# Expert products two units ahead: the order of first products, weight parts and relu in a decay attention and mixture-of-experts kernel

## The reference

```
out = decayed linear attention of q, k, v          # (2, 8, 768, 64)
x   = out as 1536 tokens of 512 features
e   = argmax(x @ w_gate);  gate = softmax(...)[e]
for each expert e, for its own tokens xe:
    y = gate * (relu(xe @ w1[e]) @ w2[e])
h = y @ w_in;  result = (h - tanh(h)) @ w_out
```

## Time and profile before

| | |
|---|---|
| median of 3 runs | 547.7 us (543.15 to 550.82) |
| profiled execution | 547.09 us, span 545.2 us, mean TensorE clock 0.983 |
| TensorE busy | 509.8 us, 94% of the span |
| VectorE, ScalarE, GpSimd busy | 367.3, 257.4, 319.4 us |
| chain that ended last | TensorE 85%, VectorE 4%, DMA 4%, issue 3%, ScalarE 2%, GpSimd 1% |
| DMA | 64.55 MB, mean 118 GB/s |

### The profile page before, as it was taken

One profiled execution on the slowest core, in us unless ns is written; L12 is line 12 of the kernel. 1 busy time (PEld: TensorE's weight loads), 2 busy tenths in 40 slices (PEclk: granted clock), 3 DMA queues, 4 the chain that ended last, 5 costly groups with the idle time before them and its releaser, 6 DMA issues.

```text
span 545.2 us, 10842 instructions
## 1 busy us (share of the span) xinstructions
PE 509.8 (94%) x3948; PEld 452.5 (83%) x3949; DVE 367.3 (67%) x513; ACT 257.4 (47%) x467; POOL 319.4 (59%) x263
## 2 busy tenths in 40 slices
PE   5999748799999999999999999999999999999994
PEld 4899648799999999999888888888888888888883
DVE  7333266756546455364379999989987774998781
ACT  1222316466656566476455454545444434443431
POOL 4766046635454444445368988986855554875553
PEclk9999969899999999999999999999999999999998
DMA  8878426465667757767280000000100000100002
GB/s 312 319 274 291 164 66 200 155 204 175 234 206 215 232 189 231 215 206 232 74 298 1 1 0 1 1 1 20 59 0 1 1 1 0 60 20 1 0 1 77
DMA packets 32410, 64.55 MB, mean 118 GB/s; under 512 B 3697, under 2 KB 7793, under 8 KB 32369
## 3 DMA queue, kind: packets, MB, share of 16 engines
q1 hardware_dynamic: 30448, 57.71, 32.2%
q0 software_dynamic: 1920, 6.29, 3.5%
HBM read 57.69 MB, written 6.29 MB: 117 GB/s over the span
## 4 chain that ended last, share of the span: by engine, by line
PE 85%; DVE 4%; DMA 4%; issue 3%; ACT 2%; POOL 1%; SPq 1%; ACTq 0%; DVEq 0%; POOLq 0%
PE bank L318 25%; PE bank L320 25%; PE bank L319 24%; DMA wst<-in_w_dram 3%; PE bank L1156 2%; PE bank L1131 2%; PE bank L1142 2%; PE bank L1178 1%; PE bank L1242 1%; PE bank L1185 1%; PE bank L1168 1%; DVE x_sorted L1031 1%; POOL out_dram L650 1%; ACT x_h L742 1%; DMA x_sorted<-token_rows,tokid 1%
## 5 line engine op out<-in xcount | busy, mean ns | idle before, releaser
L608 POOL TENSOR_TENSOR w_l<-wst,w_h 128x512 fp32r<-128x512 f32 x64 | 84.5, 1321 | 105.7 <-ACT w_h L713 105.7
L658 POOL TENSOR_SCALAR big<-h_sq 128x512 uint8<-128x512 f32 x48 | 80.3, 1673 | 37.3 <-ACT h_sq L797 37.0
L671 POOL TENSOR_TENSOR g_l<-g,g_h 128x512 fp32r<-128x512 f32 x48 | 63.9, 1330 | 45.5 <-ACT g_h L807 45.5
L318 PE MATMUL bank<-wo_h,g_h 128*128 128x512 f32 x192 | 75.4, 393 | 0.0
L320 PE MATMUL bank<-wo_l,g_h 128*128 128x512 f32 x192 | 75.1, 391 | 0.0
L319 PE MATMUL bank<-wo_h,g_l 128*128 128x512 f32 x192 | 74.6, 389 | 0.0
L320 PE MATMUL bank<-x_l,win_h 128*128 128x512 f32 x188 | 74.3, 395 | 0.0
L318 PE MATMUL bank<-x_h,win_h 128*128 128x512 f32 x188 | 73.9, 393 | 0.0
L319 PE MATMUL bank<-x_h,win_l 128*128 128x512 f32 x188 | 73.7, 392 | 0.0
L318 PE MATMUL bank<-xs_h,w_h 128*128 (+1 forms) x256 | 70.9, 277 | 2.6 <-issue 1.4
L318 PE MATMUL bank<-h_h,w_h 128*128 128x232 f32 x256 | 71.6, 280 | 1.5 <-DVE h_l L1021 1.3
(11 more groups left out here) (159 smaller groups left out, 1098.5 us busy)
## 6 DMA issues: line engine op xcount, KB each, us to landing
wst<-in_w_dram SPq DMA_DIRECT2D x128, 256.0 KB, 3.9
qk_in<-in_qk_t_dram SPq DMA_DIRECT2D x12, 512.0 KB, 6.1
kv_in<-in_kv_dram SPq DMA_DIRECT2D x12, 512.0 KB, 5.2
win<-in_w_in_dram SPq DMA_DIRECT2D x8, 512.0 KB, 4.5
wo<-in_w_out_dram SPq DMA_DIRECT2D x8, 512.0 KB, 8.0
token_rows<-x_sb SPq DMA_DIRECT2D x12, 256.0 KB, 3.4
x_sorted<-token_rows,tokid POOLq DMA_INDIRECT x12, 4.6
out_dram<-rows,tokid POOLq DMA_INDIRECT x12, 3.0
```

Of the source, the lines that this page charges most:

```text
L318: pe.matmul(dst, lh, rh, start=start, stop=False, skip_group_check=True)
L608: pool.tensor_tensor(w2_l[:, j % STG], wst2[:, j % STG], w2_h[:, j % 2].bitcast(F32), ALU.subtract).then_inc(w2l_ready, 1)
L658: pool.tensor_scalar(big[:, f % 2], h_sq[:, f % 2], T * T, None, ALU.is_ge).then_inc(big_ready, 1)
L671: pool.tensor_tensor(g_l[:, f % 2], g[:, f % 2], g_h[:, f % 2].bitcast(F32), ALU.subtract).then_inc(gl_ready, 1)
```

## The change

TensorE now runs F two units ahead: F(0) and F(1) come before the loop, and at each j the order is F(j+2), then in expert 0 the tiles of that j, then S(j). At j = 6 and 7 F belongs to the next expert, and the wait for all tiles and pads of expert 0 stands at j = 6.

On ScalarE the high part of w1 comes ahead of relu, with a wait for F(j) of its own. relu waits also for S(j-2), which read the h_h buffer. On VectorE the low part of w1 comes ahead of h_l. Tiles 2 to 11 are spread over six values of j: (2, 3), (4, 5), (6), (7, 8), (9, 10), (11); before over seven: (2, 3), (4), (5, 6), (7), (8, 9), (10), (11).

```diff
-    LATER = [[t for t in range(2, NT) if (t - 2) * (JT - 1) // (NT - 2) == j] for j in range(JT)]
+    LATER = [[t for t in range(2, NT) if (t - 2) * (JT - 2) // (NT - 2) == j] for j in range(JT)]
...
             def hidden(j, unit):
                 act.wait_ge(first_done, unit + 1)
+                ge(act, second_done, unit - 1)
                 act.activation(h_h[:, j % 2], bank[:, j % 4, 0:WIN], ACT.Relu).then_inc(hh_ready, 1)
...
                 for j in range(JT):
                     unit = JT * e + j
+                    if not (last and j + 2 >= JT):
+                        act.wait_ge(first_done, unit + 1)
+                        w1_high(j + 2, unit + 2, arrived(e, j + 2))
                     hidden(j, unit)
                     if first:
                         scale(LATER[j])
-                    if not (last and j + 2 >= JT):
-                        w1_high(j + 2, unit + 2, arrived(e, j + 2))
...
                     unit = JT * e + j
+                    if not (last and j + 2 >= JT):
+                        w1_low(j + 2, unit + 2)
                     hidden(j, unit)
                     if first:
                         scale(LATER[j])
-                    if not (last and j + 2 >= JT):
-                        w1_low(j + 2, unit + 2)
...
                 for j in range(JT):
-                    if j + 1 < JT:
-                        first_product(off, j + 1, JT * e + j + 1)
+                    if j + 2 < JT:
+                        first_product(off, j + 2, JT * e + j + 2)
                     elif not last:
-                        if first:
-                            pe.wait_ge(xsl_ready, NT)
-                            pe.wait_ge(pad_ready, 2)
-                        first_product(offset(e + 1), 0, JT * e + JT)
+                        if j + 2 == JT:
+                            if first:
+                                pe.wait_ge(xsl_ready, NT)
+                                pe.wait_ge(pad_ready, 2)
+                            off = offset(e + 1)
+                        first_product(off, j + 2 - JT, JT * e + j + 2)
...
             first_product(0, 0, 0)
+            first_product(0, 1, 1)
```

## The result

The changed kernel takes 576.65 us (median of 4 runs, 573.15 to 585.57), the kernel before 548.23 in the same comparison. The ratio is 1.057 (95% interval 1.050 to 1.063): slower. Ratios here leave out executions in the chip's slower state, such as the one of 585.57. The forecast was 571, with a range from 558 to 584.

The account below looks back on a forecast made before the run. TensorE was taken to bound the expert and last stages. Losses of 14.7, 10.8, 2.1, 1.0 and 1.2 us, less 1.6 and 4.4, gave +23.8 on 547.09: 571 us, range 558 to 584.

Parts of the forecast that it names:

- What bounds it: Expert and last stages are both set by TensorE, so only its gaps can be won; the last stage is untouched.
- The 4.4 us: Gaps at j = 1 and 2 in six later experts, from relu queued behind w1's DMA wait: all 4.4 us won.
- Term 1: F of j = 3, experts 1 to 7: w1's load behind win's comes about 2.1 us late each, 14.7 us.
- Term 2: F of j = 6 (expert 0: j = 7): win_l ahead of w1's low part, 1.35 each, 10.8 us.
- Term 4: The end: S(63) late because w2's high part waits for S(61) with one product as cover, 1.0 us.
- Term 3: GpSimd's w2 low part holds VectorE's w1 low part: 0.1 us at three units in each of seven experts, 2.1 us.
- Restarts: TensorE's slower product behind each of 15 new gaps, 0.08 us each, 1.2 us.
- Term 5: Expert 0: tile 8's wait and slow clock shrink, two late units cost 0.85 each; -1.6 us, between -4.5 and +1.5.
- The clock: Rival: the clock falls at the seven 2 us gaps, adding 11 us, so 582 us; 12 in 100.
- Rival 1: The gap is paid once, not in every expert, since later loads run far enough ahead: 546 us; 7 in 100.
- Rival 2: Either win_l's delay or the load's delay behind win hides, the other not: 560 or 564 us; 18 in 100.
- Rival 4: Ordinary loads land later than 2.9 us, 0.3 more at three units in eight and win's load: 579 us; 8 in 100.

Follow-up runs that it names:

- four moves: Changed kernel with w1's load one unit further ahead, win's high part and x_h before w2's high part, expert 0's tile takes one j later: 551.8 us, ratio 1.014.
- takes late: Changed kernel with expert 0's turned tiles taken one j later on ScalarE and VectorE, behind w1's parts and ahead of relu or h_l: 572.9 us, ratio 1.049.
- the load ahead: Changed kernel with w1's load issued one unit further ahead, in front of w2's, so win's load comes behind w1 of j = 3: 567.2 us, ratio 1.041.
- five moves: Changed kernel with the four moves and also w2's low part made by VectorE behind h_l instead of by GpSimd: 553.4 us, ratio 1.017.

## Why the prediction was right

**What bounds it** held: the loss is in the expert stage, in gaps of TensorE, the restarts behind them and products at half clock.

**The 4.4 us** were won. No second product starts late for its h; those late follow a slow product, and S(63) is its own case.

**Term 1** (14.7) measured 13.8, in seven gaps from 1.23 to 2.97. That it is win's load was shown by moving it alone. That the sum came so close is partly luck: from w2's issue to w1's high part it took 6.18 us on the mean of experts 2 to 7, not 5.73, and the four products had about 0.4 us more than 5.36, by the small gap and the restarts at j = 2. **Term 2** (10.8) measured 9.4, eight gaps of 1.07 to 1.35; moving win's high part alone took most of it away. **Term 4** (1.0) measured 0.88. **Term 3** (2.1) was mis-sized: the gaps outside j = 3 and 6 at full clock sum to some 4.2, 0.3 each at j = 0 and 2 and 0.1 each at j = 5. The mechanism was right (w_l 932 to 686 ns without GpSimd), but the chain is 2.98, not 2.88 (S(20)'s end at 162.91 to F(24) at 165.89; the last step, from w_l's end to F, took 0.25 and not 0.14), and the whole 0.3 falls on each of the two units, j = 0 and 2. **Restarts** (1.2) measured 3.1, with 38 restarts behind S(7), not 15: each small gap has one too.

**Term 5** (-1.6) is where the prediction failed in sign: expert 0 is 1.9 us slower, one F more taken off. The long wait for tile 8 and its slow clock are gone, 3.5 and 1.6 us, more than the 1.7 and 1.6 that were counted. But all six gaps showed (1.0 to 1.16 each), not two, since without that wait nothing hid four of them. They are 1.16 and not 0.85 where two tiles are taken: one take on ScalarE was counted, but there are two (0.96 us, 87.67 to 88.63), and then VectorE's two xs_l of 0.6 us each end last ahead of w1's low part. With one tile, before F(5), the gap is 1.00. Another 1.3 of the 1.9 is the clock: F(0) took 2.71 us, at half clock. The kernel before had such a stretch too, a mean clock of 0.50 from 76 to 79 us, ahead of its stage. The four kernels with the takes in the same place and no slow start needed 34.6 to 34.9 us for expert 0, 0.2 to 0.5 more than before with the F taken off. Against them, moving the takes took 3.3 to 3.6 us off.

**The clock** was a rival (12 in 100) and came in two experts of seven: 3.4 us, not 11. The forecast of full clock throughout the stage was wrong. Sum: 13.8 + 9.4 + 4.2 + 0.9 + 3.1 + 3.4 + 1.9 - 4.4 = 32.3, the stage's 221.3 less 189.0. 2.0 were won ahead of it, which no term holds: the start of F(0) lies between 80.6 and 83.9 us in the fourteen kernels. The forecast of 23.8 was low by the restarts (1.9), the clock (3.4) and expert 0 (3.5); terms 1 and 2, a little high, and term 3, low, cancel but for 0.3.

**Rival 1** (the gap is paid once) is excluded: it came in every expert. **Rival 2** is too: both kinds of gap are there. **Rival 4** came only for the load behind win, with up to 7.04 us; at j = 1, 4 and 7 no gap of F at full clock was seen.

## What to carry to other kernels

Running a producer further ahead lengthens the time from product to its use and shortens, by as much, the time from a freed buffer to the next load's deadline; count both distances in units of the bound engine before moving it. Where an engine waits for data that sits behind one late transfer, move the transfer first: that won all 4.4 us that the reordering was for, and no new gap came. A large gap covers others on the same path, so the gain of removing it is smaller than it is long.

## What the runs showed of the hardware

In the changed kernel 1.99 us in which TensorE stood, before F(27), were followed by 3.5 us at a mean granted clock of 0.51, mostly the 1.2 GHz level, and 2.80 us, before F(19), by none: the following product took its usual 1.41, and the clock from 150.6 to 154 us was 1.00.

```profile
150.60:154.00 3.40, 3.37 (x29) 3.40 (x30) 2.22 (x4) 1.97 (x4) 1.29 (x1) 1.00 0.21 71
```

Length alone does not tell; what does stays open.

VectorE's scaling of a tile, one source and one scalar, usually takes 0.48 us. It took longer than 1 us eleven times in the fourteen kernels: 4.59 before, 3.12 with four moves, 2.22 with takes late, 1.30 to 2.19 elsewhere. Each time GpSimd was in a subtraction when the scaling began, or in a gather with a subtraction right behind it, and each time the scaling ended 0.27 to 0.30 us after GpSimd's subtractions and memsets had paused (103.52 behind 103.23, 98.00 behind 97.70). So its length was that of what GpSimd still had to do without a pause. One shorter case does not fit whole: a scaling of 0.77 us with the load ahead ended 0.29 behind a memset, though a subtraction followed at once. In the two kernels where GpSimd makes no subtraction beside it (w2's low part on VectorE, five moves) every scaling took 0.48.
